# Expert loop of a routed layer: tiles of 32 tokens in four column groups instead of tiles of 128

## The reference, cut to what matters

```python
do_compute = x @ w_skip > 0                       # about half the tokens
e_idx = argmax(x @ w_gate)                        # one expert each
for e in range(8):
    mask = e_idx == e
    h = np.maximum(xc[mask] @ w1[e], 0.0)         # 384 -> 1024
    y[mask] = gate_w[mask, None] * (h @ w2[e])    # 1024 -> 384
out[do_compute] = xc + y
```

## Time and profile before

| | |
|---|---|
| median of 3 runs | 431.92 us (430.95 to 433.26) |
| profiled execution, its time | 430.86 us |
| profiled execution, its span | 429.1 us |
| mean granted PE clock | 0.981 |
| expert loop | 182.9 to 351.0 us of the span |
| busy over the span | PE 91%, PE weight load 71%, DVE 61%, ACT 38%, POOL 24% |

### The profile page before, as it was taken

The page is one execution under the profiler, slowest core; times in us unless marked ns, Lnnn a source line. Parts: engine busy times, 40 slices in busy tenths (PEclk is TensorE's granted clock), DMA queues, the critical chain, the costliest instruction groups (busy, mean ns, idle before and its releaser), DMA issues.

```text
span 429.1 us, 10101 instructions
## 1 busy us (share of the span) xinstructions
PE 390.1 (91%) x3912; PEld 305.5 (71%) x3913; DVE 262.4 (61%) x547; ACT 161.9 (38%) x464; POOL 103.4 (24%) x133
## 2 busy tenths in 40 slices
PE   0799999999999999899999999999999998999861
PEld 0578877777777887777788888888888887855340
DVE  8999999999999346544444444444445354851042
ACT  1567887787678642011111111111111112831031
POOL 2214424443443500312222222222222220020000
PEclk9979999999999999999999999999999998999997
DMA  8957556756779994111485958586767737599929
GB/s 319 388 183 281 217 198 245 249 191 217 256 237 350 397 409 194 38 37 38 171 330 194 324 203 316 216 299 234 279 244 269 259 108 251 215 392 390 373 98 361
DMA packets 40977, 106.97 MB, mean 249 GB/s; under 512 B 3552, under 2 KB 23264, under 8 KB 40432
## 3 DMA queue, kind: packets, MB, share of 16 engines
q1 hardware_dynamic: 38704, 99.62, 62.9%
q0 software_dynamic: 2240, 6.88, 4.7%
HBM read 88.80 MB, written 17.69 MB: 248 GB/s over the span
## 4 chain that ended last, share of the span: by engine, by line
PE 51%; DMA 9%; DVE 6%; issue 1%; ACT 1%; DVEq 0%; POOLq 0%; POOL 0%; ACTq 0%
PE a_bank L611 20%; PE y_bank L622 19%; DMA e_sb<-in_moe_w 4%; DMA x_sb<-in_moe_w 3%; PE a_bank L649 3%; PE a_bank L532 2%; DVE x_sb L1170 1%; PE y_bank L638 1%; DMA results<-ys,put_now 1%; DMA work<-tokens,take_i 1%; DMA back<-results 1%; PE a_bank L669 1%; DVE k_in L955 1%; PE sums_bank L540 1%; ACT bonus_v L790 1%
## 5 line engine op out<-in xcount | busy, mean ns | idle before, releaser
L611 PEld LDWEIGHTS a_bank<-batch_t,w_sb 128*128 128x128 f32 x768 | 88.2, 192 | 5.3 <-issue 1.3
L611 PE MATMUL a_bank<-batch_t,w_sb 128*128 128x128 f32 x768 | 88.4, 275 | 1.1 <-issue 1.1
L1100 DVE STREAM_TRANSPOSE work<-parts 32x96 f32<-32x96 f32 x256 | 69.1, 270 | 28.0 <-DMA parts<-tokens,take_now 24.7
L622 PE MATMUL y_bank<-w_sb,work 128*128 128x384 f32 x256 | 85.2, 486 | 0.0
L1193 POOL TENSOR_SCALAR_AFFINE_SELECT a_sb<-a_sb 128x512 f32<-128x512 f32 x48 | 50.7, 1058 | 86.5 <-ACT a_sb L780 86.5
L622 PEld LDWEIGHTS y_bank<-w_sb,work 128*128 128x128 f32 x256 | 47.4, 190 | 29.7
L856 ACT ACTIVATE work<-a_bank 128x512 f32<-128x512 f32 x32 | 19.1, 597 | 130.8 <-PE a_bank L611 130.8
L1105 DVE COPY ys<-y_bank 128x384 f32<-128x384 f32 x16 | 8.9, 558 | 68.2 <-PE y_bank L622 68.2
L790 ACT ACTIVATE bonus_v<-v_sb,bonus 128x48 f32<-128x48 f32 x192 | 44.9, 327 | 0.0
L469 PE MATMUL a_bank<-r_in,k_in 64*128 64x128 f32 x384 | 36.9, 314 | 1.5 <-DVE r_in L956 0.5
L469 PEld LDWEIGHTS a_bank<-r_in,k_in 64*128 64x128 f32 x384 | 27.2, 200 | 11.7 <-issue 6.7
(11 more groups left out here) (234 smaller groups left out, 480.9 us busy)
## 6 DMA issues: line engine op xcount, KB each, us to landing
w_sb<-in_moe_w SPq DMA_DIRECT2D x20, 1536.0 KB, 10.7
wrk_sb<-in_wrk SPq DMA_DIRECT2D x16, 768.0 KB, 7.3
e_sb<-in_moe_w SPq DMA_DIRECT2D x8, 1536.0 KB, 14.8
wrk_sb<-in_wrk SPq DMA_DIRECT2D x15, 780.0 KB
v_sb<-in_vt SPq DMA_DIRECT2D x16, 288.0 KB, 2.8
results<-work SPq DMA_DIRECT2D x1, 4608.0 KB, 15.1
tokens<-x_sb SPq DMA_DIRECT2D x4, 1152.0 KB, 14.1
x_sb<-in_moe_w SPq DMA_DIRECT2D x3, 1536.0 KB, 15.4
```

The source lines that it names most:

```text
L611: last = nc.tensor.matmul(bank[2 + f // 4][:, (f % 4) * P:(f % 4 + 1) * P], w1_sb[j][:, kk, f * P:(f + 1) * P], x_t[:, kk, :], start=(kk = ...
L622: last = nc.tensor.matmul(bank[4][:, 0:DM], h_t[:, f, :], w2_sb[j][:, f, :], start=(f == 0), stop=(f == FK - 1))
L1100: last = V.transpose(turned_rows[SQ * o:SQ * (o + 1), :, SQ * i:SQ * (i + 1)], rows_by_block[SQ * i:SQ * (i + 1), :, SQ * o:SQ * (o + 1)])
```

## The change

Each expert now gets a whole number of tiles of 32 tokens. Four such tiles form a group of 128 rows, which is gathered and put as one tile was before; a group may hold rows of two experts. The tiles are 7, 8, 5, 7, 7, 7, 5 and 5, together 51, and the last group is filled up, so that 52 are run in 13 groups.

In a tile the tokens are the stationary operand in both products. First product: for each of three channel parts four products, one to each column group, with 32 columns of tokens and 256 columns of `w1` streaming; the hidden values of the tile come out on 4 x 32 partitions by 256. ACT takes the relu to `hid`, DVE turns it in blocks of 32x32 to `h_t`. For this `w2` is reordered on the host, so that each partition's rows are one run. Second product: for each of four blocks, four products of 192 columns; column groups 0 and 1 hold one half of the sum over hidden values, 2 and 3 the other. ACT copies both halves out (`y_low`, `y_high`), DVE adds them into the tile's 32 rows of `ys`. The rows for `x_t` are brought over by four copies, two on ACT and two on DVE (`take_x`).

The order on PE is: first product of tile k + 1, second product of tile k. SP's loads wait for the second product instead of the put. The loop is written out for each expert, and PE reads nine counts ahead of it.

```diff
+            ends = [pe.value_load(tiles_i[0:1, e:e + 1], ...) for e in range(E + 1)]
+            idle_products(23)
+            def first_layer(j):
+                for kk in range(DK):
+                    for g in range(PER):
+                        last = nc.tensor.matmul(bank[2][SUB * g:SUB * (g + 1), 0:FB], x_t[:, kk, :], w1_sb[j][:, kk, FB * g:FB * (g + 1)],
+                                                start=(kk == 0), stop=(kk == DK - 1), tile_position=(0, SUB * g), skip_group_check=True)
+                last.then_inc(h_full, 1)
+            def second_layer(j):
+                for b in range(FK // 2):
+                    for g in range(PER):
+                        k, d = FK // 2 * (g // 2) + b, YW * (g % 2)
+                        last = nc.tensor.matmul(bank[4][SUB * g:SUB * (g + 1), 0:YW], h_t[:, SUB * k:SUB * (k + 1)], w2_sb[j][:, k, d:d + YW],
+                                                start=(b == 0), stop=(b == FK // 2 - 1), tile_position=(0, SUB * g), skip_group_check=True)
+                last.then_inc(ffn_done, 1)
...
+                    with pe.Fori(first + 1, end) as t:
+                        pe.wait_ge(xt_ready_act, t + 1)
+                        pe.wait_ge(xt_ready_dve, t + 1)
+                        pe.wait_ge(h_ready, t)
+                        first_layer(j)
+                        pe.wait_ge(ht_ready, t)
+                        pe.wait_ge(y_parts_ready, t)
+                        second_layer(j)
...
 ACT
+                for s in range(PER):
+                    act.wait_ge(h_full, PER * g + s + 2)
+                    if s == PER - 2:
+                        act.wait_ge(rows_turned, g + 2)
+                    take_x((s + 2) % PER)
+                    act.wait_ge(ht_ready, PER * g + s + 1)
+                    relu_hidden()
+                    act.wait_ge(ffn_done, PER * g + s + 1)
+                    act.wait_ge(ys_added, PER * g + s + 1)
+                    nc.scalar.activation(y_low, bank[4][0:2 * SUB, 0:YW], ACT.Copy)
+                    nc.scalar.activation(y_high, bank[4][2 * SUB:, 0:YW], ACT.Copy).then_inc(y_parts_ready, 1)
...
 DVE
+                for s in range(PER):
+                    dve.wait_ge(h_full, PER * g + s + 2)
+                    if s == PER - 2:
+                        dve.wait_ge(rows_turned, g + 2)
+                    take_x((s + 2) % PER)
+                    if s == PER - 3:
+                        ...
+                        dve.wait_ge(ld_rows_in, 16 * g + 32)
+                        turn_rows()
+                    dve.wait_ge(h_ready, PER * g + s + 2)
+                    dve.wait_ge(ffn_done, PER * g + s + 1)
+                    turn_hidden()
+                    dve.wait_ge(y_parts_ready, PER * g + s + 2)
+                    if s == 0:
+                        dve.wait_ge(results_stored, 16 * g + 16)
+                    for d in range(2):
+                        rows = slice(SUB * d, SUB * (d + 1))
+                        last = V.tensor_tensor(ys[SUB * s:SUB * (s + 1), YW * d:YW * (d + 1)], y_low[rows, :], y_high[rows, :], ALU.add)
+                    last.then_inc(ys_added, 1)
...
 POOL
+                wait(rows_turned, g + 2)
+                ...
+                take_rows()
+                wait(ys_added, PER * g + PER + 1)
+                nc.gpsimd.tensor_copy(put_now[:, :], put_i[:, bass.ds(g, 1)]).then_inc(index_ready, 1)
+                wait(index_ready, 2 * g + 4)
+                put_rows()
...
 SP
-                sp.wait_ge(results_stored, over)
+                sp.wait_ge(ffn_done, end)
```

More of the change, by code:

```diff
@@ L405, in _ @@
                     load_e2(sp, 3)
+            sp.wait_ge(results_stored, over)
             for q in range(NT // 2):
@@ L594, in _ @@
             last.then_inc(inverse_full, 1)
[L595 to L598, removed]
+            idle_products(2)
             pe.wait_ge(routed, 1)
[L600 to L613, removed]
[L614 to L624 removed]
@@ L629, in _ @@
+            pe.wait_ge(h_ready, ends[E] + 1)
             idle_products(32)
@@ L861, in _, with take_x, relu_hidden @@
-            act.wait_ge(xt_ready, total + 1)
+            def take_x(s):
+                for o in range(PER // 2):
+                    last = nc.scalar.activation(x_t[SUB * o:SUB * (o + 1), :, :],
+                                                turned[SUB * s:SUB * (s + 1), :].rearrange("p (k o t) -> p k o t", o=PER, t=SUB)[:, :, o, :],
+                                                ACT.Copy)
+                last.then_inc(xt_ready_act, 1)
+            def relu_hidden():
+                nc.scalar.activation(hid[:, :], bank[2][:, 0:FB], ACT.Relu).then_inc(h_ready, 1)
@@ L1107, in _, with turn_rows, take_x, turn_hidden @@
-            fetched = dve.snap(16 * total + 16)
+            def turn_rows():
+                V.transpose(turned, rows_in).then_inc(rows_turned, 1)
+            def take_x(s):
+                for o in range(PER // 2, PER):
+                    last = V.tensor_copy(x_t[SUB * o:SUB * (o + 1), :, :],
+                                         turned[SUB * s:SUB * (s + 1), :].rearrange("p (k o t) -> p k o t", o=PER, t=SUB)[:, :, o, :])
+                last.then_inc(xt_ready_dve, 1)
+            def turn_hidden():
+                V.transpose(h_t, hid[:, :]).then_inc(ht_ready, 1)
@@ L1108, in _ @@
+            fetched = dve.snap(16 * groups + 32)
             dve.wait_ge(ld_rows_in, fetched)
@@ L1277, in pack, with by_quarters @@
     return wrk, vt, ublock.reshape(P, -1)
+def by_quarters(w):
+    import numpy as np
+    E, F, DM = w.shape
+    return np.ascontiguousarray(w.reshape(E, 4, F // 128, 32, DM).transpose(0, 1, 3, 2, 4).reshape(E, 128, -1))
 def kernel(**inputs):
```

174 lines of the change are left out of this document (93 added, 81 removed).

## The result

The changed kernel takes **470.58 us** (median of 4 runs, 465.54 to 473.77); the kernel before took 431.44 beside it (4 runs, 430.81 to 433.26). The ratio is 1.086, interval 1.076 to 1.096; it compares the means without the run of 473.77, which counts as slow. The change made the kernel slower, as forecast, but by 39 us where 16 were forecast, which is above the range.

What follows compares the result with a forecast made beforehand. It took the expert loop's two products, 39% of the span, as the bound. Loop with landings +3.9, clock +6.5, start +5.3, tables -0.2 and end +0.7 made +16.2: 448 us, slower, range 422 to 462.

Steps and rivals of the forecast that it cites:

- Layers at 1.30 us: PE's two products in a tile: 1.30 us for each layer, 2.60 us a tile, 135.2 us for 52 tiles.
- Just inside 2.6: Chain in a tile from first product through ACT's copies and relu to the next: 2.4 us, fitting under PE's 2.6.
- tile chain: Rival: costlier 32-partition copies make ACT's chain pace PE at 3.0 us a tile; +10, 458 us; chance 0.13.
- A group of 11.87: Four tiles with idle put: 6.67 us from E (PE's last second product issued) to next first product, plus 5.2 of layers.
- Landings, 17.4: Puts in the loop issued behind weight loads land later than 2.70 us; six of them add 17.4 us, bounds 0 and 41.
- The clock, five falls of 1.3: PE's clock falls after the 4.6 to 4.9 us pauses in five groups, 1.3 us each: +6.5, bounds 0 and 8.5.
- Start, +5.3: Before the loop, nine reads (5.4 us), 23 idle products (5.2) and a fallen clock put the first product at 188.2.
- End, +0.7: At the loop's end the last rows are complete 1.45 us after PE's last issue instead of 0.76: +0.7 us.
- Code loading: Rival: PE's longer written-out loop needs seven more code blocks and waits for them; +7 to +30, 455 to 478 us; chance 0.10.
- No wait: Rival: no add in the loop waits on a put, so the pauses vanish; 406.6 us; chance 0.04.
- hidden: Weight loads in the loop cost nothing: a pair lands 11.1 us after issue, the shortest expert lasts over 13.
- Puts land fast: Rival: all puts land in 2.7 us, pauses are 1.5 us and the clock stays; 424.2 us, faster; chance 0.14.

Runs made afterwards that it cites:

- Experiments 1 and 9: Against the changed kernel: 1, two `ys` tiles taken in turn by group, 418.08 us; 9, one `ys` tile, each quarter put by its own transfer, 418.76 us.
- Experiment 8: The kernel of experiment 7 with one of ScalarE's two copies of the turned rows in each tile made by VectorE; 410.88 us.
- experiment 11: The changed kernel with only one of ScalarE's two copies of the turned rows in each tile moved to VectorE; 472.28 us.
- experiment 6: The changed kernel with `w2` padded by 16 floats in each piece of a row, so that runs are 1.5 KB; 470.05 us.
- Experiment 5: The changed kernel with TensorE's tile loops written out and 20 idle products ahead of each first product that waits for a put; 478.38 us.
- experiments 3 and 4: Against the changed kernel: 3, no loads in the loop, loop 171.3 us instead of 199.0; 4, TensorE's tile loop written out, 478.18 us.
- experiment 7: The kernel with two `ys` tiles, each of TensorE's nine reads followed by two idle products and none behind the last; 413.44 us.

## Why the prediction was too low

The main mechanism was right: the add at the head of a group waits for the whole put (twelve times), TensorE stands behind VectorE's queued copy, late puts go with the loads, the clock falls behind the late ones. Experiments 1 and 9 settle the cause, each in its own way: take the wait away with a second buffer or with puts of a quarter, and 52 us go. What failed is the sum, five of whose terms were too small: groups and ends by 8.6 us, late landings by 7.3, the clock by 4.6, the end by 2.8 and the start by 1.5. Two of these hide an error of mechanism: a put that was counted as outside the loads, and blocks of code beside puts.

- *Layers at 1.30 us:* right. Experiment 8 runs tiles at 2.60.
- *"Just inside 2.6":* the first step of the working that failed. First product to first product measured 1.50 + 0.05, two copies 0.57, 0.03, relu 0.38, 0.15: 2.68, not 2.4. The copies were 0.57 where I took 0.4, and the two signals about 0.2 where I took 0.1. So ScalarE paces the tiles at 2.68 to 2.74; by the Trainium skill, "TensorEngine Tiling", section Performance Considerations, copies out of PSUM may bind once the product is fast. The trace agrees in part: ScalarE's chain binds by 0.08 us and more in a tile, but only the relu in it (0.38) reads PSUM; the two copies (0.57) read `work`. The rival "tile chain" thus held in its mechanism. Its price in this kernel is small: the four layers behind a put take 5.52 instead of 5.20 (0.32 in a group), and experiment 11 shows that moving the copy gives nothing back.
- *A group of 11.87:* 12.48. E to first product is 6.88 to 6.98 instead of 6.67 (the put is issued at E + 2.90 to 3.00, not 2.77), the layers behind it 5.52. With the ends 8.6 us in all, the largest miss.
- *Landings, 17.4:* 24.7. The four puts behind fresh sets took 6.3 to 7.6, where I took 6.15 from the rows of before (+3.5); in experiment 6, with the short runs of before, they took 6.0 to 6.4. The put after tile 40 (345.38) was counted as outside, but the loads behind tile 41 were issued 0.15 us before it (345.23), and it took 7.0 (+4.4). That was in the forecast's own counts: the loads 2.6 us after E, the put 2.8. The put after tile 36 was counted with 3.1 more and had 0.4; those after 32 and 44 had 2.1 more than counted, each with a block of code beside it. Without loads 4.3 are left, which go with blocks of code. The bounds (0 and 41) held.
- *The clock, five falls of 1.3:* seven falls, 1.1 to 2.2 each, 11.1 in all, above the upper bound of 8.5. I took the length of a low stretch (3.4 us) from the row with a pause of 1.9 us. The five behind the landings of 6.3 and more were low for about 6.8 us and cost 8.5. The other two, behind pauses of 2.1 and 3.3 us, were low for 3.4 and cost 2.6; I had not counted on a fall there. Experiment 5 shows that this part is the clock. The Trainium skill, "TensorE: Matmul & The Clock Gate", section HAM oscillation, warns of kernels that pause for a transfer each round; the trace agrees in seven of the twelve pauses, and not in the five of 1.4 to 1.8 us.
- *Start, +5.3:* the reads took 5.4, as forecast. The clock was put on the first product (1.3), but the 23 idle products bore it, 7.1 instead of 5.2. It was put down to the pause of the reads, but it had fallen 1.2 us before that pause began; in experiment 8 it did not fall there at all. Why it falls at this place is open. The first product is at 189.5, not 188.2.
- *End, +0.7:* 3.5. In the tail TensorE stands 1.85 and 2.55 us for `e_sb` (1.82 and 2.39 before); the second time the clock then fell, which it had not before, and the small products behind it run at 1.2 GHz for some 6 us; 2.7 of the 3.5 us arise behind the first of these waits. Why it fell this time only is open.
- *Code loading:* 6 more blocks, near the seven forecast, and PE did not wait for them. But blocks fell on the puts, which the forecast did not have (experiments 3 and 4).
- *"No wait", 406.6:* experiment 1 is that case, with 418.1. Its difference is made of much the same misses: 1.3 at the start, 52 tiles x 0.14 = 7.3, weights 2.4; sum 417.6. That the weights are "hidden" was wrong there: with no pauses the loop is fast enough to meet them.
- *"Puts land fast", 424.2:* did not come; even there the 8.6 of the groups and the 4.3 of start and end would have made it 437, slower than before.

What stays open: how a block of code of 16 KB makes a put 2 us later, and why not each time (in experiment 5 one put with a block beside it landed in 2.6); what makes the clock fall ahead of the loop; and how much of a landing under load is due to the position in the set and how much to the length of its runs. The gather was not tried by itself.

## What to carry to other kernels

When several small steps are batched into one transfer, the buffer that it empties needs a second copy, or the transfer must stay as fine as the writes; else the first write of the next batch waits for the whole transfer, and every engine that is held by that write waits too. Price such a wait with the landing under the loads that run beside it, place each transfer against the loads by what triggers the two, and add the low clock behind it, for all of the low stretch. Before moving work from one engine to another, see which chain the receiving engine's queue is part of: the same edit was worth 2.6 us with the wait gone and nothing with it.

## What the runs showed of the hardware

- TensorE's nine reads of a value take 0.6 us each, and only 1.4 us of them ran under products queued ahead. With idle products put between them, the clock, which had fallen before the reads in experiment 7, rose again while they went on.
- In the changed kernel's loop the granted clock fell in pauses of 5.2 to 6.4 us to 0.50, and it stayed there for 6.8 us, of which 3 to 5.2 were work; behind pauses of 2.1 and 3.3 us it was there for 3.4; behind pauses of 1.4 to 1.8 us it did not fall. With the long pauses filled by idle products it stayed at 1.00.
- A put of 192 KB landed in 2.6 us with empty queues, 6.3 to 7.6 behind 4.6 MB of loads, and 4.2 to 4.9 four times with one 16 KB block of code and no load beside it. A put of 48 KB landed in 2.2 us at best and 7.5 at worst: a quarter of the bytes saves little.
- Two loads of 1.5 MB took 11.8 us with puts, gathers and one block of code beside them, 0.6 MB in all.
- A 32x96 copy took 281 ns on ScalarE and 245 on VectorE, not much less than 64x192 takes on ScalarE (324), with four times the elements.
